# Products 0 to 3 in one row, then six tiles: the units of the second MLP in another order

## The reference

```python
mu = np.mean(x, axis=-1, keepdims=True)
var = np.mean((x - mu) ** 2, axis=-1, keepdims=True)
xn = (x - mu) / np.sqrt(var + 1e-06) * g_ln
ch = np.maximum(xn @ w_ch1, 0.0) @ w_ch2
return (x + ch).astype(np.float32)
```

## Time and profile before

| | |
|---|---|
| median of 3 runs | 464.21 us (462.81 to 464.45) |
| profiled execution | 462.69 us, its span 461.0 us |
| granted TensorE clock | 1.00 in every slice, the 2.4 GHz level |
| TensorE matmuls | 452.0 us busy, 98% of the span |
| VectorE | 277.4 us, 60% |
| ScalarE | 200.7 us, 44% |
| GpSimd | 268.2 us, 58% |

### The profile page before, as it was taken

One profiled execution on the slowest core, in us unless ns is written; L12 is line 12 of the kernel. 1 busy time (PEld: TensorE's weight loads), 2 busy tenths in 40 slices (PEclk: granted clock), 3 DMA queues, 4 the chain that ended last, 5 costly groups with the idle time before them and its releaser, 6 DMA issues.

```text
span 461.0 us, 8619 instructions
## 1 busy us (share of the span) xinstructions
PE 452.0 (98%) x3114; PEld 400.7 (87%) x3114; DVE 277.4 (60%) x630; ACT 200.7 (44%) x503; POOL 268.2 (58%) x405
## 2 busy tenths in 40 slices
PE   7899999999999999999999999999999999999997
PEld 6677788989989889989899989998999899889985
DVE  4999976876666977974674633557562234233333
ACT  4898997433335746435333145314221232133210
POOL 2559689999945000097888865880032687888000
PEclk9999999999999999999999999999999999999999
DMA  9998961212102000002115333211120211220003
GB/s 220 217 219 187 197 164 55 92 47 91 47 0 93 0 1 0 1 0 91 48 47 139 113 61 101 91 46 47 46 92 0 93 39 54 91 93 0 1 0 137
DMA packets 74725, 35.28 MB, mean 77 GB/s; under 512 B 57632, under 2 KB 68924, under 8 KB 74684
## 3 DMA queue, kind: packets, MB, share of 16 engines
q1 hardware_dynamic: 71164, 33.85, 26.8%
q10 hardware_dynamic: 3520, 0.88, 0.9%
HBM read 28.83 MB, written 3.15 MB: 69 GB/s over the span
## 4 chain that ended last, share of the span: by engine, by line
PE 92%; DMA 3%; SPq 2%; DVE 1%; POOL 1%; issue 0%; ACT 0%; DVEq 0%; POOLq 0%
PE two L1699 10%; PE two L1698 10%; PE two L1697 9%; PE two L1674 9%; PE two L1677 9%; PE two L1676 8%; PE two L1470 5%; PE two L1472 5%; PE two L1471 5%; PE two L1605 5%; PE two L1606 5%; PE two L1604 5%; PE two L1455 2%; PE two L1434 2%; PE two L1423 2%; PE two L1352 1%
## 5 line engine op out<-in xcount | busy, mean ns | idle before, releaser
L639 POOL TENSOR_TENSOR asum<-wst 128x256 f32<-128x256 f32 x26 | 21.5, 829 | 95.5 <-PE two L1472 50.2
L1674 PE MATMUL two<-combo,wa 128*128 128x384 f32 x224 | 75.5, 337 | 0.1
L1677 PE MATMUL two<-combo,wa 128*128 128x384 f32 x224 | 75.4, 337 | 0.0
L1699 PE MATMUL two<-wv,h 128*128 128x512 f32 x192 | 75.3, 392 | 0.0
L1698 PE MATMUL two<-wv,h 128*128 128x512 f32 x192 | 75.2, 392 | 0.0
L1676 PE MATMUL two<-combo,wa 128*128 128x384 f32 x224 | 75.2, 336 | 0.0
L1697 PE MATMUL two<-wv,h 128*128 128x512 f32 x192 | 74.7, 389 | 0.0
L1274 ACT ACTIVATE h<-u 128x384 fp32r<-128x384 f32 x32 | 16.8, 525 | 74.7 <-DVE u L1012 67.3
L633 POOL TENSOR_TENSOR wa<-asum,wa 128x256 fp32r<-128x256 f32 x52 | 44.9, 863 | 4.3
L573 POOL TENSOR_SCALAR pn<-ex,rinv 128x120 f32<-128x120 f32 x96 | 34.7, 381 | 19.4 <-DVE rinv L735 18.7
L1470 PE MATMUL two<-xT,win 128*128 128x384 f32 x128 | 43.6, 341 | 0.0
(11 more groups left out here) (119 smaller groups left out, 944.1 us busy)
## 6 DMA issues: line engine op xcount, KB each, us to landing
wst<-in_moe_w_ch SPq DMA_DIRECT2D x26, 512.0 KB, 3.2
vW<-in_v SPq DMA_DIRECT2D x13, 288.0 KB
kn<-in_k SPq DMA_DIRECT2D x15, 192.0 KB, 3.5
qn<-in_q SPq DMA_DIRECT2D x15, 192.0 KB, 3.8
out<-y SPq DMA_DIRECT2D x11, 256.0 KB, 2.0
wst<-in_moe_w_in SPq DMA_DIRECT2D x8, 256.0 KB, 3.1
wst<-in_moe_w_out SPq DMA_DIRECT2D x8, 256.0 KB, 2.9
tok<-xq SPq DMA_DIRECT2D x32, 48.0 KB, 2.0
```

Of the source, the lines that this page charges most:

```text
L1674: nc.tensor.matmul(o, wk[:, 0, kk], ck[:, 0, kk], start=(first and kk == 0), stop=False, skip_group_check=True)
L1677: ins = nc.tensor.matmul(o, wk[:, 1, kk], ck[:, 0, kk], start=False, stop=(kk == 1), skip_group_check=True)
L1699: ins = nc.tensor.matmul(o, lo, vh, start=False, stop=(f == NFP - 1 and c == 1), skip_group_check=True)
```

## The change

In units 1 to 14 TensorE runs p0 p1 p2 p3, all six tiles of the unit before, then p4 p5 p6. Units 0 and 15 keep their order on TensorE. VectorE's other work stands in every unit between u3 and c22. In all 16 units c21 now stands ahead of low1. The scaling of the second half of the turned tokens moves from unit 5 to unit 6, its DMAs from behind load 5 to behind load 6, and the combinations are now made as 0 to 3 (unit 7) and 4 to 6 (unit 8).

```diff
--- before.py
+++ after.py
@@ -65,7 +65,7 @@
 
 
         TOK_TILE = {11: {0: 0, 1: 1, 3: 2, 4: 3}, 12: {0: 4, 1: 5, 3: 6, 4: 7}}
-        TOK_UNIT = {4: range(4), 5: range(4, 8)}
+        TOK_UNIT = {4: range(4), 6: range(4, 8)}
         NSLOT = 2 * KD
 
 
@@ -508,8 +508,8 @@
             for l in range(NLOAD):
                 load_a(l)
                 load_v2(l)
-                if l in (4, 5):
-                    move_tokens(l - 4)
+                if l in (4, 6):
+                    move_tokens((l - 4) // 2)
                 if l == NFP:
                     for n in range(T):
                         store(n)
@@ -976,12 +976,6 @@
             dve.wait_ge(hg_done, 2 * KF)
             for g in range(NU):
                 a, b = ps_h[g % 2][:, 0:HALF], ps_h[1 - g % 2][:, 0:HALF]
-                if g == 2:
-                    inverse_std(1)
-                    dve.wait_ge(rstd_done, 2)
-                    for i in range(3):
-                        centre(1, i)
-                        turn_blocks(i)
                 dve.wait_ge(p1_done, g + 1)
                 if g >= 1:
                     dve.wait_ge(h2_done, 4 * g)
@@ -989,53 +983,46 @@
                 nc.vector.tensor_tensor(u2[:], b, p1[:], ALU.add).then_inc(u2_done, 1)
                 if g == NFP + 1:
                     add_out(5)
+                h2_low(g, 0)
+                dve.wait_ge(prod_done, NPROD * g + 4)
+                nc.vector.tensor_tensor(u3[:], b, p1[:], ALU.add).then_inc(u3_done, 1)
+
+
+                if g == 1:
+                    for i in range(T):
+                        stats(T + i)
+                elif g == 2:
+                    inverse_std(1)
+                    dve.wait_ge(rstd_done, 2)
+                    for i in range(3):
+                        centre(1, i)
+                        turn_blocks(i)
+                elif g == 4:
+                    for i in range(3, T):
+                        centre(1, i)
+                        turn_blocks(i)
+                elif g == 6:
+                    token_sums(1, (0, 1, 2))
                 elif g == NFP - 1:
                     token_sums(1, (3,))
-                h2_low(g, 0)
-                if g == 1:
-                    for i in range(4):
-                        stats(T + i)
-                elif g == 6:
-                    token_sums(1, (0, 1))
-                elif g == NFP - 1:
-                    for k in range(3):
+                    for k in range(4):
                         combo_low(1, k)
                 elif g == NFP:
-                    combo_low(1, 5)
-                    combo_low(1, 6)
-                    add_out(0)
-                    add_out(1)
-                dve.wait_ge(prod_done, NPROD * g + 4)
-                nc.vector.tensor_tensor(u3[:], b, p1[:], ALU.add).then_inc(u3_done, 1)
+                    for k in range(4, NPROD):
+                        combo_low(1, k)
+                    for n in range(5):
+                        add_out(n)
                 dve.wait_ge(prod_done, NPROD * g + 5)
                 dve.wait_ge(u3_done, g + 1)
                 nc.vector.tensor_tensor(u3[:], a, u3[:], ALU.add).then_inc(c22_done, 1)
-                h2_low(g, 1)
-                if g == 1:
-                    for i in range(4, T):
-                        stats(T + i)
-                elif g == 3:
-                    for i in (3, 4):
-                        centre(1, i)
-                        turn_blocks(i)
-                elif g == 6:
-                    token_sums(1, (2,))
-                elif g == NFP - 1:
-                    combo_low(1, 3)
-                    combo_low(1, 4)
-                elif g == NFP:
-                    for n in range(2, 5):
-                        add_out(n)
                 dve.wait_ge(prod_done, NPROD * g + 6)
                 nc.vector.tensor_tensor(c21[:], b, p1[:], ALU.add).then_inc(c21_done, 1)
+                h2_low(g, 1)
                 dve.wait_ge(prod_done, NPROD * g + 7)
                 dve.wait_ge(u2_done, g + 1)
                 nc.vector.tensor_tensor(u2[:], a, u2[:], ALU.add).then_inc(c12_done, 1)
                 h2_low(g, 2)
                 h2_low(g, 3)
-                if g == 3:
-                    centre(1, 5)
-                    turn_blocks(5)
             for n in range(T, NTT):
                 add_out(n)
 
@@ -1314,15 +1301,15 @@
                 nc.scalar.copy(p1[:], a[:, 0:HALF]).then_inc(p1_done, 1)
                 if g == 0:
                     copy_y(T)
-                elif g == NFP:
-                    combo_high(1, 5)
-                    combo_high(1, 6)
                 h2_high(g, 0)
                 if g == 0:
                     for n in range(T + 1, T + 4):
                         copy_y(n)
                 elif g == NFP - 1:
-                    for i in range(3):
+                    for i in range(4):
+                        combo_high(1, i)
+                elif g == NFP:
+                    for i in range(4, NPROD):
                         combo_high(1, i)
                 for slot in slots:
                     tokens(1, slot, tok[:, slot // KD, slot % KD])
@@ -1337,9 +1324,6 @@
                         copy_y(n)
                 elif g == 1:
                     root(1)
-                elif g == NFP - 1:
-                    combo_high(1, 3)
-                    combo_high(1, 4)
                 h2_high(g, 2)
                 h2_high(g, 3)
 
@@ -1709,13 +1693,15 @@
                     contract(g - 1, i)
 
             for g in range(NU):
-                for k in range(3):
+                whole = 0 < g < NU - 1
+                for k in range(4 if whole else 3):
                     product(g, k)
-                for i in range(3):
+                for i in range(T if whole else 3):
                     tile(g, i)
-                product(g, 3)
+                if not whole:
+                    product(g, 3)
                 product(g, 4)
-                if g < NU - 1:
+                if g == 0:
                     for i in range(3, T):
                         tile(g, i)
                 product(g, 5)
```

## The result

The changed kernel takes 465.69 us (median of 12 runs, 464.71 to 466.81) and the one before 463.98 us (12 runs, 462.81 to 465.85). The profiled execution took 465.53 us, its span is 463.8 us (before 462.69 and 461.0), and the granted TensorE clock is 1.00 in both. The prediction's words for this outcome were a small loss of 1 to 3 us, and "same" with a chance of 0.56.

A forecast was written before the change was run, and what follows sets the result against it. TensorE, busy for 452.0 of 461.0 us, was taken as the bound. Terms of 0.4, 0.9, 0.5 and 0.35 us, given as 2.1, were added to 463.5, the mean of four executions: 465.6 us, range 463.2 to 468.6.

The forecast's parts named there:

- Bound: Whole kernel: MLP2 runs as fast as TensorE takes its matmuls; reordering can only remove existing stalls or add new ones.
- c22 and c21: Units 1 to 14, p4 to p6 in a row: c22 and c21 still come in time, cost 0.
- u2 at clean seams: Before p3 in units 1 to 14: slack falls to 0.19, costing 0.03 us a unit, 0.4 us in all.
- u2 when VectorE is late: Before p3: u2's lateness from low halves stretched beside GpSimd, formerly hidden by three tiles, now reaches p3; 0.9 us.
- low1 between c21 and c12: Unit seams: where GpSimd is in an instruction, low1 waits it out and c12 with it; 0.5 us in sum.
- The square root: Behind high1 of unit 1: ScalarE's table load and root delay copy p1, so product 2 stalls once by 0.35 us.
- Token DMAs: 16 DMAs move behind one more pair of loads, ending in unit 5; scaling moves to unit 6; cost 0.
- Signs: New profile: product 3's loads idle, released by u2; low1 stretched at seams of units 3 to 5; table load between high1 and high2.
- Rival 2: Low halves meet GpSimd at every seam, 0.37 us a unit in 12 units, 4.4 us; total 468.7 us; chance 0.19.

The follow-up runs named there:

- e_pe_only: Kernel before with only TensorE's new order; VectorE, ScalarE and SyncE keep the old order: 489.19 us, ratio 1.0553, two runs.
- e_small_after: Changed kernel with GpSimd's instructions from batch 3 on cut to 4 columns instead of 256 or 512, all waits kept: 463.27 us, ratio 1.0008.
- e_shift: Changed kernel with GpSimd's instructions cut to 4 columns from batch 3 on, plus four small VectorE instructions in unit 9: 463.93 us, one run.
- e_low1_last: Changed kernel with low1 moved behind c12: 473.53 us, ratio 1.0202, four runs.
- e_best: Changed kernel with three tiles before p3, low1 behind c12, root before high1, some VectorE work including one unit 2 centring before u3: 463.38 us, ratio 1.0004.
- e_unit0: Kernel before with low1 behind c12 in unit 0 only, instead of ahead of c21: 463.08 us, ratio 0.9990.

## Why the prediction was right, step by step

- **Bound.** Right. TensorE is busy for 97 or 98% of the span in all of these kernels but e_pe_only (95%), and no order gained a measurable time.
- **c22 and c21, cost 0.** Right: at +0.19 or +0.20 of their products in all of units 1 to 14, and no wait of p4 to p6 shows.
- **u2 at clean seams, 0.4.** Too high. In clean units the seven products do take 7.40 us where they took 7.36 (unit 13 of both), which is close to the 0.03 a unit of the working. But the unit stays at 15.60, so the six tiles, now in one row, take 8.20 instead of 8.24. The term left out what the other side of the move gives back; net it is 0.
- **u2 when VectorE is late, 0.9.** The mechanism is right, the size was off: 1.6. The lateness of before was carried over as it stood, but the new places of low2 and low3 met GpSimd in other units (4, 6 and 2 instead of 3, 12 and 14). And 0.3 of it, unit 11, was put down to GpSimd in error: it is the hitch in VectorE's own stream, as e_small_after and e_shift showed.
- **low1 between c21 and c12, 0.5.** The mechanism is right, the size was off: 0.9, plus 0.4 at product 2 behind the copy p1, less 0.21 for the old stall. That step had seen c12, but not that high3 stands ahead of the copy and carries the delay on. The stall at the seam of units 4 and 5, where GpSimd was to be at work once its load had moved, came as 0.31 (0.2 predicted); that of units 3 and 4 did not come at c12, but one product later at u2, 0.34.
- **The square root, 0.35.** It is 0.09, and 0.1 to 0.15 where nothing else held that unit up. The copy starts 0.53 behind product 1, where the working had about 0.8 (3.9 against 3.1): ScalarE's instructions behind one another start some 0.4 apart, and the working gave high2 and high3 0.5 to 0.55 each.
- **Token DMAs, 0.** Right, and the 7.21 us of GpSimd's idle time are gone.
- **Signs.** u2 is named as the releaser, and the table load stands between high1 and high2. low1 is stretched at the seams of units 4 and 5 (1.14) and 5 and 6 (0.87), not at that of 3 and 4 (0.55).

The sum was 2.1 us; the profile shows 2.8 (spans and stretches agree), and the medians 1.7. The errors partly cancelled: 0.4 and 0.3 too much for clean seams and the root, and at the seams where a sum comes late 1.2 too little (1.6 + 0.9 + 0.4 - 0.2 = 2.7, less 0.1 that is the root's, is 2.6, where 0.9 + 0.5 = 1.4 stood). That the forecast of 465.6 us lies 0.1 from the median is luck in part: the kernel before came out at 463.98 instead of the 463.5 that the sum started from, and the loss by medians was 0.4 under the 2.1. Rival 2, a loss of 4.4 at every seam, has the mechanism but not the frequency; it is what e_low1_last made real, with 8.6 us in 11 units. As for the rule of the Trainium skill (SBUF — State Buffer, "SBUF: two separate sides"), by which one engine waits for the whole instruction of the other: the traces agree: low halves took 1.08 to 1.23 us where 0.56 is alone, the sum c12 with an input in PSUM kept 0.54 beside a GpSimd sum, and with shorter GpSimd instructions the stretching went.

## What to carry to other kernels

When work moves on the engine that is the bound, list for every wait the cover that it loses, and then look at who else can delay the engine that is waited for: a slack of 0.2 us is free when that engine is on time and lost whenever it shares something with a third one. Follow a delay one step further than the first wait, as here from low1 over c12 and high3 to the copy. A stall that comes back in the next run belongs to the order, and an edit elsewhere can move it or its gain away, as in e_best and e_unit0; so test a small gain on the whole kernel and not on the seam.

## What the runs showed of the hardware

- **VectorE and GpSimd take turns.** A low half of 0.56 us (two operands from SBUF) took 1.08 to 1.23 when GpSimd was in an instruction as it began, and three in a row took a turn each. Sums with one input in PSUM kept 0.54 to 0.56. It goes both ways: GpSimd's 0.41 us instruction of line 631 took 0.59 and its 0.74 us sums 0.92 to 1.08 (in units 1 to 5 of the changed kernel).
- **A hitch of 0.36 us in VectorE's stream**, in unit 11, in kernels with either order, with GpSimd busy or nearly idle; with four more instructions ahead of it, in the one run tried, it was gone.
- **The clock falls after idle time.** In e_pe_only TensorE, busy for 0.63 of 3.99 us, was granted 0.50 of its clock over the second product after that, the 1.2 GHz level; in the changed kernel stalls of 0.3 to 0.5 us left it at 1.00, and in e_low1_last stalls of up to 1.1 us left it at 0.999.
